# Six of seven groups of streamed tiles begin at other remainders of 256 bytes

## The chip, the cores and the metric

The kernel runs on one core of one Trainium2 chip. The metric is the device time of one launch in microseconds (us). Before the change the median of two runs is 1595.04 us (1594.94 to 1595.14).

## The reference, cut to what matters

There are four batches of 3136 positions. An attention without softmax is followed by a small gated convolution layer, all in float32:

```
scores = (z @ z.T) / 3136                 # z: 3136 x 64
attn   = relu(scores) ** 2
x      = u * (attn @ v)                   # v, u: 3136 x 256
h      = relu(x @ w_in)                   # w_in: 256 x 1024
conv   = sum over k of conv_w[k] * h shifted by k-1 positions, k = 0, 1, 2
out    = (h * sigmoid(conv)) @ w_out      # w_out: 1024 x 256
```

## The kernel before, in words

**Number format.** Every product is made of three matmuls. Each operand is split into a rounded part (`_hi`, in the format that TensorE takes for four-byte operands) and the rest (`_lo`), and hi by hi, lo by hi and hi by lo are summed in PSUM. ScalarE writes each `_hi` tile by a copy, VectorE writes each `_lo` tile by a subtraction, both in the same layout.

**Two kinds of operands.** A matmul has a stationary operand, loaded 128 columns at a time by a weight load (`z_hi`, `z_lo`, `v_hi`, `v_lo`, `w_hi`, `w_lo`), and a moving operand, which streams through the array column by column. Seven groups of tiles stream: `z_mv` (the positions of a block, hi and lo, for the scores), `attn_hi` and `attn_lo` (for attn @ v), `x_hi` and `x_lo` (for x @ w_in), `g_hi` and `g_lo` (for the last product). Every weight load and every matmul of the blocks works on 64 of the 128 partitions, so matmuls come in pairs, one on the upper and one on the lower half, that run side by side. Only the products of the last block use all 128.

**Blocks.** 28 blocks, seven per batch. A block is 448 positions wide in the first three batches, and 512, 512, 512, 448, 448, 448 and 256 in the last. In each block PAIRS = 13 steps go over the keys. A step issues on TensorE, in an order written out by hand: attend for one pair of key tiles (line 481, in two halves), a piece of the up or down product of the block before (lines 503 and 527), the scores three steps ahead (line 397; lines 429, 434 and 437 for the last key tile of a block). Each matmul has its own weight load. The tables USUAL and NARROW say at which step each piece of the layer after the attention is made. The last block's layer stands alone at the end (lines 547 and 567), and the last two blocks keep their gated tiles in the space of `v_hi` and `v_lo`.

**Widths.** Scores, attend and up products stream the block's own width. The down product streams 450 columns in the last block of the first three batches and 258 in the last of all, where the convolution's border belongs to the block.

**Addresses.** Every tensor is laid at a multiple of LINE = 256 bytes. The seven moving groups have SHIFT = 16 elements of four bytes in front, so their first column is 64 bytes past such a multiple. Their rows are PITCH = 512 elements (2048 bytes) apart, so every row begins at the same remainder. The gated tiles in `v_hi` and `v_lo` keep the same 64 bytes (lines 272 to 276), except that the last block's second rows lie 288 elements (1152 bytes) on and so begin at remainder 192. All stationary tiles begin at multiples of 512 bytes. `h_sb`, which VectorE and ScalarE read and write, has rows of 516 elements, so its rows begin at eight different remainders, 16 bytes apart.

**Around the matmuls.** ScalarE makes the first relu of a score tile (line 649), rounds `attn_hi` (658), `x_hi` (675) and `g_hi` (724), and forms `h_sb` (698). VectorE squares (834), subtracts for `attn_lo` (855), `x_lo` (885), `g_lo` (916) and the low half of `z_mv` (934), and makes two taps of the convolution (895, 903). The loads and stores are issued on SyncE's queue and none of them touches a moving tile.

Of the kernel before, what the change touches and what calls it, by code (L numbers as in the profile page):

```python
# [6 lines left out]
F32R = mybir.dt.float32r  # L7
# [3 lines left out]
P = 128  # L11
# [9 lines left out]
PITCH = 512  # L21
# [10 lines left out]
AHEAD = 3  # L32
LINE = 256
SHIFT = 16

RAW = 512
RING = 6
# [81 lines left out]
def program(nc, z_win, z_all, v_all, u_win, w_all, conv_w, out):  # L119
    with ExitStack() as ctx:  # L120
        def sb(name, shape, dt=F32):
            return ctx.enter_context(nc.sbuf_tensor(name, shape, dt, align_bytes=LINE))

        def shifted(name, rows, columns):
            return sb(name, [P, SHIFT + rows * columns], F32R)[:, SHIFT:].rearrange("p (r k) -> p r k", r=rows)

        def sem(name):
            return ctx.enter_context(nc.semaphore(name))
# [1 line left out]

        z_hi = sb("z_hi", [P, PAIRS * P], F32R)
        z_lo = sb("z_lo", [P, PAIRS * P], F32R)
        z_mv = sb("z_mv", [P, SHIFT + 4 * PITCH], F32R)[:, SHIFT:].rearrange("p (b r k) -> p b r k", b=2, r=2)
        z_raw = sb("z_raw", [P, WIDE])
        v_hi = sb("v_hi", [P, TILES * MODEL], F32R)
        v_lo = sb("v_lo", [P, TILES * MODEL], F32R)
# [4 lines left out]

        attn = sb("attn", [P, 3, 2, WIDE])
        attn_hi = shifted("attn_hi", 6, PITCH)
        attn_lo = shifted("attn_lo", 6, PITCH)

        u_sb = sb("u_sb", [P, CM, WIDE])
        x_sb = sb("x_sb", [P, CM, WIDE])
        x_hi = shifted("x_hi", CM, PITCH)
        x_lo = shifted("x_lo", CM, PITCH)
        h_sb = sb("h_sb", [P, FT, HWIDE])  # L150
        g_sb = sb("g_sb", [P, 2, 2, WIDE])
        g_hi = shifted("g_hi", 2, PITCH)
        g_lo = shifted("g_lo", 2, PITCH)
# [116 lines left out]
        def gated_parts(m, F):  # L270
# [4 lines left out]
            at = (FP * 2 * PITCH if m == BLOCKS - 1 else 0) + F * step  # L275
            return [part[:, at:at + step].rearrange("p (r k) -> p r k", r=2)[:, :, SHIFT:] for part in (v_hi, v_lo)]

# [838 lines left out]
```

## Time and profile before

| | us |
|---|---|
| median of the runs | 1595.04 |
| the profiled execution's own time | 1595.02 |
| its span, first to last instruction | 1593.2 |
| TensorE matmul busy | 1584.1 (99%) |
| TensorE weight load busy | 1560.5 (98%) |
| VectorE busy | 1390.5 (87%) |
| ScalarE busy | 1169.3 (73%) |
| GpSimd busy | 35.8 (2%) |

The busy time of TensorE is the time in which at least one matmul was in flight. Since several are in flight at once, the duration of one (359 ns at 448 columns) says little of the rate. The rate is read from the distance between the starts of successive matmuls in the timeline. A timeline line with x2 holds one pair (upper and lower half), a line with x4 two pairs.

### The profile page before, as it was taken

The page shows a single profiled execution, that of the slowest core. Times are in us where ns is not written, and L with a number is a line of the kernel's source. Part 1 is how long each engine was busy: PE and PEld are TensorE (multiplying, and loading weights), DVE is VectorE, ACT ScalarE, POOL GpSimd, SP SyncE. Part 2 cuts the span into 40 slices and gives each one's busy share as a digit, 9 for nine tenths or more (in the row PEclk, how much of TensorE's full clock was granted, in tenths as well). Part 3 has the DMA queues.
Part 4 walks back from the last instruction along what each step waited for, and adds up shares of the span by engine and source line. Part 5 has one row for each costly group of instructions (what it writes and reads, how often), then busy time and mean ns, then how long its engine had stood idle before and what let it go on. Part 6 is the DMA issues. An engine that isn't in the chain of part 4 may idle for free.

```text
span 1593.2 us, 37744 instructions
## 1 busy us (share of the span) xinstructions
PE 1584.1 (99%) x15604; PEld 1560.5 (98%) x15604; DVE 1390.5 (87%) x1940; ACT 1169.3 (73%) x2016; POOL 35.8 (2%) x28
## 2 busy tenths in 40 slices
PE   9999999999999999999999999999999999999998
PEld 7999999999999999999999999999999999999998
DVE  7898888899988888889998888888999888888888
ACT  7777677777777777778777677777877676777776
POOL 6200000000000000000000000000000000000000
PEclk9999999999999999999999999999999999999999
DMA  5100000111000000011200000001110000000000
GB/s 161 38 19 21 23 19 30 53 45 59 22 28 21 31 13 19 30 52 45 65 33 14 19 30 13 19 30 66 52 51 33 4 29 14 19 32 15 21 15 31
DMA packets 29770, 53.16 MB, mean 33 GB/s; under 512 B 2720, under 2 KB 19744, under 8 KB 29600
## 3 DMA queue, kind: packets, MB, share of 16 engines
q1 hardware_dynamic: 29600, 50.76, 9.8%
q8 instruction: 124, 2.03, 0.5%
q14 instruction: 46, 0.38, 0.1%
HBM read 37.89 MB, written 12.85 MB: 32 GB/s over the span
## 4 chain that ended last, share of the span: by engine, by line
PE 95%; DVE 2%; ACT 1%; issue 1%; POOL 0%; DMA 0%; SPq 0%; ACTq 0%
PE ps_av L481 50%; PE ps_h L503 16%; PE ps_y L527 16%; PE ps_s L397 12%; ACT attn_hi L658 0%; POOL v_lo L1061 0%; DVE v_lo L916 0%; DVE attn_lo L855 0%; DMA raw<-v_all 0%; PE ps_s L567 0%; ACT attn L649 0%; DVE g_sb L903 0%; DVE g_sb L895 0%; PE ps_s L429 0%; DVE attn L834 0%
## 5 line engine op out<-in xcount | busy, mean ns | idle before, releaser
L649 ACT ACTIVATE attn<-ps_s 128x448 f32<-128x448 f32 (+2 forms) x650 | 318.4, 542 | 377.5 <-PE ps_s L397 375.9
L834 DVE SCALAR_TENSOR_TENSOR attn<-ps_s,attn 128x448 f32<-128x448 f32 (+2 forms) x650 | 374.9, 618 | 124.2 <-ACT attn L649 122.4
L481 PE MATMUL ps_av<-attn_hi,v_hi 64*128 64x448 f32 (+2 forms) x2740 | 453.9, 359 | 1.1 <-DVE x_sb L879 0.8
L481 PE MATMUL ps_av<-attn_hi,v_lo 64*128 64x448 f32 (+2 forms) x2740 | 454.0, 359 | 0.3 <-POOL v_lo L1061 0.2
L481 PE MATMUL ps_av<-attn_lo,v_hi 64*128 64x448 f32 (+2 forms) x2740 | 453.3, 359 | 0.5 <-DVE attn_lo L855 0.5
L855 DVE TENSOR_TENSOR attn_lo<-attn,attn_hi 128x896 fp32r<-128x896 f32 (+3 forms) x363 | 384.5, 1059 | 55.9 <-ACT attn_hi L658 30.7
L658 ACT ACTIVATE attn_hi<-attn 128x896 fp32r<-128x896 f32 (+3 forms) x363 | 335.9, 925 | 0.1
L481 PEld LDWEIGHTS ps_av<-attn_hi,v_hi 64*128 64x128 f32 x2740 | 326.2, 184 | 5.5 <-issue 2.7
L481 PEld LDWEIGHTS ps_av<-attn_hi,v_lo 64*128 64x128 f32 x2740 | 326.2, 184 | 4.0 <-POOL v_lo L1061 1.6
L481 PEld LDWEIGHTS ps_av<-attn_lo,v_hi 64*128 64x128 f32 x2740 | 326.6, 184 | 3.4 <-DVE attn_lo L855 0.9
L397 PE MATMUL ps_s<-z_mv,z_hi 64*128 64x448 f32 (+2 forms) x1296 | 276.1, 360 | 0.0
L503 PE MATMUL ps_h<-x_hi,w_hi 64*128 64x448 f32 (+1 forms) x864 | 199.9, 363 | 0.4 <-issue 0.2
L503 PE MATMUL ps_h<-x_lo,w_hi 64*128 64x448 f32 (+1 forms) x864 | 199.7, 362 | 0.0
L503 PE MATMUL ps_h<-x_hi,w_lo 64*128 64x448 f32 (+1 forms) x864 | 199.6, 362 | 0.0
L527 PE MATMUL ps_y<-g_lo,w_hi 64*128 64x448 f32 (+2 forms) x832 | 193.8, 363 | 0.0
L527 PE MATMUL ps_y<-g_hi,w_hi 64*128 64x448 f32 (+2 forms) x832 | 193.6, 363 | 0.0
L527 PE MATMUL ps_y<-g_hi,w_lo 64*128 64x448 f32 (+2 forms) x832 | 193.5, 363 | 0.0
L397 PEld LDWEIGHTS ps_s<-z_mv,z_hi 64*128 64x128 f32 x1296 | 178.8, 184 | 2.0 <-DVE attn L834 0.7
L397 PE MATMUL ps_s<-z_mv,z_lo 64*128 64x448 f32 (+2 forms) x648 | 148.3, 359 | 0.0
L895 DVE SCALAR_TENSOR_TENSOR g_sb<-h_sb,taps,g_sb 128x448 f32<-128x448 f32 (+3 forms) x218 | 141.3, 690 | 0.0
L903 DVE SCALAR_TENSOR_TENSOR g_sb<-h_sb,taps,g_sb 128x448 f32<-128x448 f32 (+3 forms) x218 | 140.2, 685 | 0.0
L710 ACT ACTIVATE g_sb<-h_sb,taps 128x448 f32<-128x448 f32 (+3 forms) x218 | 134.4, 669 | 0.0
(133 smaller groups left out, 1898.6 us busy)
## 6 DMA issues: line engine op xcount, KB each, us to landing
raw<-v_all SPq DMA_DIRECT2D x48, 256.0 KB, 2.7
u_sb<-u_win SPq DMA_DIRECT2D x24, 448.0 KB, 3.8
out<-y_sb SPq DMA_DIRECT2D x21, 448.0 KB, 2.9
z_raw<-z_win SPq DMA_DIRECT2D x24, 224.0 KB, 3.7
raw<-z_all SPq DMA_DIRECT2D x12, 256.0 KB, 3.4
raw<-w_all SPq DMA_DIRECT2D x8, 256.0 KB, 2.9
u_sb<-u_win SPq DMA_DIRECT2D x3, 512.0 KB, 3.4
out<-y_sb SPq DMA_DIRECT2D x3, 512.0 KB, 2.6
```

Of the source, the lines that this page charges most:

```text
L397: done = mm(scores_bank(n, p)[:, e, 0:WIDTHS[n]], w[rows, at:at + P], z_mv[rows, n % 2, z, 0:WIDTHS[n]], start=k == 0, stop=k == 2)
L481: done = mm(ps_av[:, c, 0:WIDTHS[n]], v[rows, j * MODEL + c * P:j * MODEL + (c + 1) * P], a[rows, 2 * slot(n, p) + e, 0:WIDTHS[n]], start= ...
L503: done = mm(ps_h[:, e, 0:WIDTHS[m]], w[rows, at:at + P], x[rows, c, 0:WIDTHS[m]], start=k == 0 and not second, stop=k == 3 * CM - 1 and se ...
L527: done = mm(ps_y[:, c, 0:outputs(m)], w[rows, at:at + P], g[rows, e, 0:outputs(m)], start=F == 0 and e == 0 and k == 0 and not second, sto ...
L649: act.activation(attn[:, slot(n, p), e, 0:WIDTHS[n]], scores_bank(n, p)[:, e, 0:WIDTHS[n]], ACT.Relu, scale=1.0 / SEQ / SEQ).then_inc(relu ...
L658: act.activation(attn_hi[:, at:at + k, 0:WIDTHS[n]], attn[:, slot(n, p), 0:k, 0:WIDTHS[n]], ACT.Copy).then_inc(attn_rounded, 1)
L710: act.activation(gated(m, f // 2)[:, f % 2, 0:outputs(m)], h_sb[:, f, 0:outputs(m)], ACT.Copy, scale=taps[:, 0, f:f + 1]).then_inc(tap0_re ...
L834: dve.scalar_tensor_tensor(a, scores_bank(n, p)[:, e, 0:WIDTHS[n]], 0.0, a, ALU.max, ALU.mult).then_inc(attn_ready, 1)
L855: dve.tensor_tensor(attn_lo[:, at:at + k, cols], attn[:, slot(n, p), 0:k, cols], attn_hi[:, at:at + k, cols].bitcast(F32), ALU.subtract).t ...
L895: dve.scalar_tensor_tensor(g, h_sb[:, f, HALO:HALO + outputs(m)], taps[:, 1, f:f + 1], g, ALU.mult, ALU.add).then_inc(tap1_ready, 1)
L903: dve.scalar_tensor_tensor(g, h_sb[:, f, 2 * HALO:2 * HALO + outputs(m)], taps[:, 2, f:f + 1], g, ALU.mult, ALU.add).then_inc(conv_ready, 1)
```

## The change

Each moving group but `attn_hi` gets its own lead in place of the common 16 elements. In bytes: `z_mv` 48, `attn_lo` 80, `x_lo` 96, `g_hi` 160, `x_hi` 192, `g_lo` 224; `attn_hi` stays at 64. The leads are at most 64 elements long, so with the rounding to 256 bytes every tensor keeps its place and only the columns within the six tensors move. The number of instructions, their order and their waits are untouched. The gated tiles inside `v_hi` and `v_lo` still use SHIFT.

```
+SHIFTS = {"x_hi": 48, "x_lo": 24, "g_hi": 40, "g_lo": 56, "attn_lo": 20, "z_mv": 12}
...
         def shifted(name, rows, columns):
-            return sb(name, [P, SHIFT + rows * columns], F32R)[:, SHIFT:].rearrange("p (r k) -> p r k", r=rows)
+            by = SHIFTS.get(name, SHIFT)
+            return sb(name, [P, by + rows * columns], F32R)[:, by:].rearrange("p (r k) -> p r k", r=rows)
...
-        z_mv = sb("z_mv", [P, SHIFT + 4 * PITCH], F32R)[:, SHIFT:].rearrange("p (b r k) -> p b r k", b=2, r=2)
+        z_mv = sb("z_mv", [P, SHIFTS["z_mv"] + 4 * PITCH], F32R)[:, SHIFTS["z_mv"]:].rearrange("p (b r k) -> p b r k", b=2, r=2)
```

## Rows read from the trace of the kernel before

**Rows 1.** The page: busy time by engine, granted clock in 40 slices, chain by engine.

```profile
PE 1584.1 (99%) x15604; PEld 1560.5 (98%) x15604; DVE 1390.5 (87%) x1940; ACT 1169.3 (73%) x2016; POOL 35.8 (2%) x28
...
PEclk9999999999999999999999999999999999999999
...
PE 95%; DVE 2%; ACT 1%; issue 1%; POOL 0%; DMA 0%; SPq 0%; ACTq 0%
```

**Rows 2.** The page's groups: busy us, mean ns | idle before, what ended it.

```profile
L481 PE MATMUL ps_av<-attn_lo,v_hi 64*128 64x448 f32 (+2 forms) x2740 | 453.3, 359 | 0.5 <-DVE attn_lo L855 0.5
...
L397 PE MATMUL ps_s<-z_mv,z_hi 64*128 64x448 f32 (+2 forms) x1296 | 276.1, 360 | 0.0
L503 PE MATMUL ps_h<-x_lo,w_hi 64*128 64x448 f32 (+1 forms) x864 | 199.7, 362 | 0.0
...
L397 PE MATMUL ps_s<-z_mv,z_lo 64*128 64x448 f32 (+2 forms) x648 | 148.3, 359 | 0.0
```

**Rows 3.** TensorE's groups by shape, lines 527 and 437.

```profile
L527 PE MATMUL ps_y<-g_lo,w_hi 64*128 64x448 f32 x640 | 143.0, 358 | 0.0
...
L527 PE MATMUL ps_y<-g_lo,w_hi 64*128 64x450 f32 x96 | 25.7, 365 | 0.0
...
L527 PE MATMUL ps_y<-g_lo,w_hi 64*128 64x512 f32 x96 | 25.0, 389 | 0.0
...
L437 PE MATMUL ps_s<-z_mv,z_lo 64*128 64x448 f32 x24 | 8.6, 359 | 0.0
```

**Rows 4.** Timeline of TensorE, 448 columns: start us, length us, instruction.

```profile
764.17 0.46 PE L503 MATMUL ps_h<-x_hi,w_hi 64*128 64x448 f32 x2
...
765.37 0.46 PE L397 MATMUL ps_s<-z_mv,z_hi 64*128 64x448 f32 x2
...
767.17 0.66 PE L481 MATMUL ps_av<-attn_hi,v_hi 64*128 64x448 f32 x4
```

**Rows 5.** Timeline of TensorE, last pairs of a stretch of 450 columns.

```profile
422.59 0.40 PE L527 MATMUL ps_y<-g_hi,w_lo 64*128 64x450 f32 x2
422.79 0.40 PE L527 MATMUL ps_y<-g_hi,w_hi 64*128 64x450 f32 x2
423.00 0.40 PE L527 MATMUL ps_y<-g_lo,w_hi 64*128 64x450 f32 x2
423.21 0.40 PE L527 MATMUL ps_y<-g_hi,w_lo 64*128 64x450 f32 x2
```

**Rows 6.** Timeline of TensorE, 512 columns, ten pairs apart.

```profile
1306.37 0.66 PE L481 MATMUL ps_av<-attn_hi,v_hi 64*128 64x512 f32 x4
...
1308.66 0.66 PE L481 MATMUL ps_av<-attn_lo,v_hi 64*128 64x512 f32 x4
```

**Rows 7.** Timeline of TensorE, 256 columns in two stretches, ten pairs apart each.

```profile
1534.41 0.42 PE L481 MATMUL ps_av<-attn_hi,v_hi 64*128 64x256 f32 x4
...
1535.59 0.42 PE L481 MATMUL ps_av<-attn_lo,v_hi 64*128 64x256 f32 x4
...
1544.37 0.42 PE L481 MATMUL ps_av<-attn_hi,v_hi 64*128 64x256 f32 x4
...
1545.51 0.42 PE L481 MATMUL ps_av<-attn_lo,v_hi 64*128 64x256 f32 x4
```

**Rows 8.** Timeline of TensorE, last block: third, seventh and twelfth matmul of twelve.

```profile
1582.32 0.28 PE L567 MATMUL ps_s<-v_hi,w_lo 128*128 128x258 f32 x1
...
1582.80 0.28 PE L567 MATMUL ps_s<-v_hi,w_hi 128*128 128x258 f32 x1
...
1583.40 0.28 PE L567 MATMUL ps_s<-v_hi,w_lo 128*128 128x258 f32 x1
```

**Rows 9.** ScalarE's groups by shape: tiles written at one remainder, and at eight.

```profile
L649 ACT ACTIVATE attn<-ps_s 128x448 f32<-128x448 f32 x554 | 271.4, 542 | 318.5 <-PE ps_s L397 317.0 <-PE ps_s L418 1.4
...
L698 ACT ACTIVATE h_sb<-ps_h 128x448 f32<-128x448 f32 x192 | 94.3, 544 | 3.0
```

## The prediction

> **What bounds the kernel now.** I read the busy shares and the chain of waits first [rows 1]: TensorE is busy 99% of the span, the chain that ended last lies on it for 95%, and its granted clock is in the top tenth in every slice, that is, the 2.4 GHz level. The groups [rows 2] show that it hardly waits: 0.5 us ahead of the 2740 matmuls that stream attn_lo, and nothing ahead of those on z_mv and x_lo. So the time is the number of pairs of matmuls times the distance between their starts: 15604 / 2 = 7802 pairs, which at 200 ns would be 1560 us of the 1593.2. Whatever changes that distance changes the time, and whatever changes only VectorE or ScalarE changes it little.
>
> Then I read the distance in the timeline. At 448 columns, 15 pairs lie between the starts 764.17 and 767.17 [rows 4]: **200 ns a pair**, alike in three products with different tiles. At 512 columns ten pairs take 2.29 us, 229 ns each [rows 6]; at 256 columns they take 1.14 us or 1.18 us, 114 or 118 ns [rows 7]. One column at 2.4 GHz is 0.417 ns, so the columns alone would need 187, 213 and 107 ns. The excess is 13, 16 and 7 ns: it grows with the length of the stream and isn't a fixed price of a matmul. Something rations the stream by pieces of it.
>
> The third reading is the one that the forecast rests on. A stretch of 450 columns starts at the usual distance and then settles to 0.20, 0.21 and 0.21 us [rows 5]; from 422.59 to 423.21 it is 0.62 / 3 = 207 ns. Two columns more cost about **7 ns**, where two columns of array time are 0.8 ns. And 200 / 28 = 7.1 ns, where 28 is the number of 16-column pieces (64 bytes) in 448; 229 / 32 is 7.2, 114 / 16 is 7.1, and 207 / 29 is 7.1. The stream is delivered in pieces of 64 bytes, and a piece of which only two columns are wanted costs as much as a whole one.
>
> **The change, part by part.** No instruction, wait, DMA or order changes, and no tensor moves; only the first byte of six moving groups. The open point is whether those 64-byte pieces lie on fixed addresses. All streams of before begin at 64 bytes past 256, or at 192, so the trace can't say. I take it that they do, because a memory's pieces usually have places, and price it from [rows 5]. It is a choice, and its other answers are the rivals.
>
> Then a stream of 448 columns that begins 48, 80 (16), 96 (32), 160 (32) or 224 (32) bytes into its grid touches 29 pieces in place of 28, and one of 512 touches 33 in place of 32. Each costs 7 ns a pair.
>
> - attn_lo, remainder 80: 2740 matmuls [rows 2], 1370 pairs, 9.6 us.
> - z_mv, remainder 48: 1296 + 648 matmuls [rows 2], 972 pairs, and three lines of which one has 24 matmuls of 448 [rows 3], about 40 pairs more: 1012 pairs, 7.1 us.
> - x_lo, remainder 96: 864 matmuls [rows 2], 432 pairs, 3.0 us.
> - g_hi and g_lo, remainders 160 and 224: per part 640 matmuls of 448 and 96 of 512 [rows 3], three parts, (640 + 96) x 3 / 2 = 1104 pairs, 7.7 us. The 450-column ones cost nothing more: 32 bytes into a piece, 450 columns end 8 + 450 = 458 columns on, still in the 29th piece.
> - x_hi, remainder 192: a multiple of 64 bytes, nothing. The last block supports that: its first gated row begins at 64 and its second at 192, and the distance is 0.12 us in both, 0.48 us for four starts and 0.60 us for five [rows 8]. If it did cost 7 ns, 864 x 2 / 2 pairs would add 6.0 us.
> - The full-height matmuls of the last block that stream x_lo number 16: 0.1 us, left out.
> - Writes by VectorE and ScalarE at new remainders: ScalarE writes h_sb rows that begin at eight remainders 16 bytes apart in 544 ns, and attn rows at aligned places in 542 ns [rows 9]. So 0 to 2 ns an instruction. What hides it is VectorE's idle 13%, 203 us [rows 1]: even 100 ns on each of some 500 split instructions, 50 us, would leave it under TensorE; uncovered, that would be late split tiles and waits ahead of line 481. A slower TensorE gives these engines more room.
>
> Sum: 3918 pairs x 7 ns = **27.4 us**. On the profiled execution's own 1595.02 us, which is within 0.1 us of the median, that makes **1622 us**, 1.7% more. Nothing stands ready to absorb it, since TensorE is the bound throughout.
>
> Both ends of the unknown price: upward, the extra piece at the start and one at the end each count, 14 ns a pair, 55 us. Downward, the excess over the columns' own time, 13 ns at 448 [rows 4], could vanish for all six groups: 3918 + 864 pairs x 13 ns = 62 us less. I take 7, the value measured for a partly used piece in the same instruction form.
>
> **Rivals.**
>
> *The pieces are counted from the operand's own start (no effect).* Then 450 columns are 29 pieces and 448 are 28, wherever they begin: [rows 5] fit as well, and [rows 8] too. All new remainders are multiples of 16 bytes, so a grid of 16 bytes comes to the same. Time 1595 us. The change would move bytes and do nothing to the time. The Trainium skill, "SBUF — State Buffer", section "Door 1: The DMA port swizzle", says that the memory has lines of 16 bytes and that accesses pay when they cross into a new line; by that rule no stream here touches one line more, and the time stays. What no run here shows yet is that line size; the 7 ns for two more columns speaks for pieces of four such lines.
>
> *A grid of 32 bytes.* Only the remainders 48 and 80 are off it: z_mv and attn_lo, 2382 pairs, 16.7 us at the same price, 1612 us. Against it: 450 columns would be 57 half-pieces, 3.6 ns more, and I read 7.
>
> *Staggering helps (faster).* If the excess of 13 ns comes from streams, weight loads and writes of other engines meeting because all begin at like places, then different remainders might break it. For it: 256 columns show two rates, 114 and 118 ns, in stretches with the same addresses [rows 7], so meeting in time does matter to some nanoseconds. Against: the 448-column streams hold 200 ns in all products, whatever else runs. All of it back is 1533 us; half of it, 31 us, is 1564 us and about the 2% line. The Trainium skill, "TensorE: Matmul & The Clock Gate", section "Back-to-back issue gap", gives N / 2.4 + 2.5 ns for a single warm matmul, 189 ns at 448 columns; the trace's 200 disagrees. By that figure 11 ns a pair are there to be won, 53 us on the six groups.
>
> *The sequence breaks (slower by over 2%).* Now each stream ends where the next one begins, modulo 256 bytes: 448, 512 and 256 columns are whole multiples of 256 bytes. With different remainders that no longer holds between attn_hi and attn_lo, x_hi and x_lo, g_hi and g_lo. If a jump costs as much as a piece beside the extra piece itself, it is 14 ns a pair: 3918 x 14 = 55 us, 1650 us. For it: after a stretch of 450 columns, whose end is off the next start, the distance is 7 ns up. It decides from 31.9 us / 3918 = 8.1 ns a pair on, only 1.1 ns over my price, and x_hi's 6.0 us would do it too.
>
> **Numbers.** The forecast (64-byte grid, all five groups at about 7 ns, 1615 to 1632) gets 0.36; no effect 0.25; the 32-byte grid 0.05; the broken sequence 0.17; staggering 0.17. A measurement of this kernel tells about 2% from no change. The forecast's own spread puts a fifth of its 0.36 over the 2% line at 1627; of staggering's 0.17 about 0.12 lies over 2%. So faster 0.12, slower 0.17 + 0.07 = 0.24, the same 0.64. The range has to hold 8 in 10: 1572 (a third or so of staggering's gain) to 1652 (the broken sequence's 1650), which leaves out most of staggering and a few cases above.
>
> **What would show it.** In the timeline after, the distance between pairs that stream attn_lo, z_mv, x_lo and g settles to 207 ns and stays at 200 for attn_hi and x_hi, averaged over a run of them, since the rate seems to answer a few matmuls late. Attend, which is two parts attn_hi and one part attn_lo, would average 202.3 ns; scores 207; up 202.3; down 207. The 450-column stretches would not change. Matmul counts, clock and waits stay. 1595 throughout means the start doesn't matter; z_mv and attn_lo alone at 207 means 32 bytes; an effect in attn_hi's or x_hi's pairs means that it isn't the count of pieces.

## The result, and the profile after

The changed kernel takes **1608.36 us** (1608.29 to 1608.43, two runs) against 1595.04 us: ratio 1.0081, 95% interval 1.0065 to 1.0097. It is 13.3 us slower, half of the 27.4 us that the prediction's sum gave. The span of the profiled execution is 1606.5 us. The time given for a kernel is the median of its executions at the full granted clock; one execution of e15 (below), at 0.869 of it, took 1716.6 us and is left out.

The page of the changed kernel, with the same three lines as [rows 1]:

```profile
PE 1596.8 (99%) x15604; PEld 1555.6 (97%) x15604; DVE 1391.3 (87%) x1940; ACT 1169.6 (73%) x2016; POOL 35.8 (2%) x28
...
PEclk9999999999999999999999999999999999999999
...
PE 95%; DVE 2%; ACT 1%; issue 1%; POOL 0%; DMA 0%; SPq 0%; ACTq 0%
```

Counts, clock and chain are the same. VectorE and ScalarE are busy as long as before to within 1 us in all, so their writes at new remainders cost nothing that shows; TensorE has 12.7 us more. Its groups, which answer to [rows 2]:

```profile
L483 PE MATMUL ps_av<-attn_lo,v_hi 64*128 64x448 f32 (+2 forms) x2740 | 463.5, 360 | 0.6 <-DVE attn_lo L857 0.6
...
L399 PE MATMUL ps_s<-z_mv,z_hi 64*128 64x448 f32 (+2 forms) x1296 | 282.5, 361 | 0.0
L505 PE MATMUL ps_h<-x_lo,w_hi 64*128 64x448 f32 (+1 forms) x864 | 206.7, 367 | 0.0
...
L399 PE MATMUL ps_s<-z_mv,z_lo 64*128 64x448 f32 (+2 forms) x648 | 153.3, 361 | 0.0
```

No wait was added: 0.6 us ahead of attn_lo, nothing ahead of the others. The matmuls themselves come at a greater distance. A stretch of 600 us, all of it at 448 or 450 columns, gives that as a count. The columns are the stretch, its length, and for TensorE, weight loads, VectorE, ScalarE and GpSimd the busy time and the count, then clock, DMA share and GB/s. The kernel before:

```profile
200.00:800.00 600.00, 599.85 (x5991) 598.72 (x5989) 532.11 (x746) 445.02 (x766) 0.00 (x0) 1.00 0.11 36
```

The changed kernel:

```profile
200.00:800.00 600.00, 599.96 (x5945) 590.63 (x5943) 527.67 (x739) 441.65 (x760) 0.00 (x0) 1.00 0.11 35
```

600 us over half of 5991 is 200.3 ns a pair before, and over half of 5945 it is 201.9 ns after. Times 7802 pairs, the difference is 12.1 us, nearly all of the change. I use this count for every kernel below and call it the rate.

The timeline of TensorE in the changed kernel shows where in a step it lies:

```profile
301.12 0.43 PE L529 MATMUL ps_y<-g_hi,w_hi 64*128 64x448 f32 x2
...
302.35 0.62 PE L483 MATMUL ps_av<-attn_hi,v_hi 64*128 64x448 f32 x4
...
303.55 0.42 PE L505 MATMUL ps_h<-x_hi,w_hi 64*128 64x448 f32 x2
...
304.77 0.42 PE L399 MATMUL ps_s<-z_mv,z_hi 64*128 64x448 f32 x2
...
305.38 0.62 PE L483 MATMUL ps_av<-attn_hi,v_hi 64*128 64x448 f32 x4
```

Six pairs on g take 1.23 us (205 ns each), six of attend 1.20 us (200), six on x 1.22 us and three on z_mv 0.61 us (203), where [rows 4] has 200 for attend, up and scores.

One cycle, read to 10 ns, can't tell a nanosecond a pair. So here is the mean over all matmuls of 448 columns that start between 200 and 1150 us: the distance from a start to the next start on the same row half, by product, in ns.

| | attend | up (x) | scores (z_mv) | down (g) |
|---|---|---|---|---|
| kernel before | 200.1 | 200.0 | 200.2 | 200.1 |
| changed kernel | 200.6 | 203.0 | 202.4 | 203.7 |

With 4110 pairs of attend (2740 x 3 / 2), 1296 of up, 1012 of scores and 1104 of down, that is 2.1 + 3.9 + 2.2 + 4.0 = 12.2 us, an estimate that gives the 448-column rate to all widths. Attend, for which I had priced the largest term, pays 2 us.

### The profile page after: what moved, and what is told of

It is laid out like the page before. It is cut to its first block, busy times and chain, and to the rows that moved or that the text cites. A ratio compares the mean times of both kernels' runs of the same rounds, so it can differ in the third digit from the quotient of the medians.

```text
span 1606.5 us, 37744 instructions
## 1 busy us (share of the span) xinstructions
PE 1596.8 (99%) x15604; PEld 1555.6 (97%) x15604; DVE 1391.3 (87%) x1940; ACT 1169.6 (73%) x2016; POOL 35.8 (2%) x28
## 4 chain that ended last, share of the span: by engine, by line
PE 95%; DVE 2%; ACT 1%; issue 1%; POOL 0%; DMA 0%; SPq 0%; ACTq 0%
PE ps_av L483 50%; PE ps_h L505 17%; PE ps_y L529 16%; PE ps_s L399 12%; ACT attn_hi L660 0%; POOL v_lo L1063 0%; DVE v_lo L918 0%; DMA raw<-v_all 0%; DVE attn_lo L857 0%; PE ps_s L569 0%; ACT attn L651 0%; DVE g_sb L905 0%; DVE g_sb L897 0%; PE ps_s L439 0%; PE ps_s L436 0%
## 5 line engine op out<-in xcount | busy, mean ns | idle before, releaser
L483 PE MATMUL ps_av<-attn_hi,v_hi 64*128 64x448 f32 (+2 forms) x2740 | 463.4, 360 | 1.0 <-DVE x_sb L881 0.8
L483 PE MATMUL ps_av<-attn_lo,v_hi 64*128 64x448 f32 (+2 forms) x2740 | 463.5, 360 | 0.6 <-DVE attn_lo L857 0.6
L483 PE MATMUL ps_av<-attn_hi,v_lo 64*128 64x448 f32 (+2 forms) x2740 | 461.8, 359 | 0.2
L483 PEld LDWEIGHTS ps_av<-attn_hi,v_hi 64*128 64x128 f32 x2740 | 334.7, 184 | 8.9 <-issue 2.5
L483 PEld LDWEIGHTS ps_av<-attn_hi,v_lo 64*128 64x128 f32 x2740 | 333.6, 184 | 7.1 <-POOL v_lo L1063 1.5
L483 PEld LDWEIGHTS ps_av<-attn_lo,v_hi 64*128 64x128 f32 x2740 | 333.0, 184 | 6.7 <-DVE attn_lo L857 0.9
L399 PE MATMUL ps_s<-z_mv,z_hi 64*128 64x448 f32 (+2 forms) x1296 | 282.5, 361 | 0.0
L505 PE MATMUL ps_h<-x_lo,w_hi 64*128 64x448 f32 (+1 forms) x864 | 206.7, 367 | 0.0
L505 PE MATMUL ps_h<-x_hi,w_lo 64*128 64x448 f32 (+1 forms) x864 | 205.7, 365 | 0.0
L529 PE MATMUL ps_y<-g_hi,w_lo 64*128 64x448 f32 (+2 forms) x832 | 199.4, 366 | 0.0
```

The source lines that it names most:

```text
L399: done = mm(scores_bank(n, p)[:, e, 0:WIDTHS[n]], w[rows, at:at + P], z_mv[rows, n % 2, z, 0:WIDTHS[n]], start=k == 0, stop=k == 2)
L483: done = mm(ps_av[:, c, 0:WIDTHS[n]], v[rows, j * MODEL + c * P:j * MODEL + (c + 1) * P], a[rows, 2 * slot(n, p) + e, 0:WIDTHS[n]], start= ...
L505: done = mm(ps_h[:, e, 0:WIDTHS[m]], w[rows, at:at + P], x[rows, c, 0:WIDTHS[m]], start=k == 0 and not second, stop=k == 3 * CM - 1 and se ...
L529: done = mm(ps_y[:, c, 0:outputs(m)], w[rows, at:at + P], g[rows, e, 0:outputs(m)], start=F == 0 and e == 0 and k == 0 and not second, sto ...
```

## The experiments

**Is there a grid of 64 bytes?** Four kernels, in which only the leads differ. In the first three all seven groups share one; in the fourth the six lie on the grid, at 128 or 192 bytes, and attn_hi stays at 64.

```
-SHIFT = 16
+SHIFT = 20      # e1: 80 bytes. e2: 24 (96 bytes). e3: 0
...
 # e4, with SHIFT = 16
+SHIFTS = {"x_hi": 48, "x_lo": 32, "g_hi": 32, "g_lo": 48, "attn_lo": 32, "z_mv": 48}
```

> All seven moving groups begin at remainder 80, attn_hi included; nothing else differs from the kernel before. Fixed 64-byte places, priced from the change itself (13.3 us over 3918 pairs, 3.4 ns a pair): every one of some 7600 pairs of 448, 512 or 256 columns touches one piece more, so 26 us, 1621 us (at the 7 ns of the prediction 53 us, 1648 us). Jumps between different starts: there are none, as before, so 1595 us. If 64 itself is a favoured remainder, anything above 1595.

> All seven moving groups begin at remainder 96. Fixed 64-byte places: as at 80, 1621 us (or 1648). A grid of 32 bytes: 1595 us while 80 is slow. Jumps between different starts: none, 1595 us.

> All seven moving groups begin at remainder 0, where the stationary tiles begin too. Fixed 64-byte places: 1595 us, since 0 lies on the grid. Jumps: 1595 us. If the common start with the weight loads costs anything, it is over 1595 here alone.

> The six groups begin at different remainders that all lie on the 64-byte grid: z_mv 192, attn_lo 128, x_lo 128, g_hi 128, x_hi 192, g_lo 192, attn_hi 64. Fixed 64-byte places: no stream touches a piece more, 1595 us. Jumps between different starts: of the order of 3000 pairs follow one on another remainder; if these made the 13.3 us of the change (4.4 ns each), the time is about that of the change, 1608 us.

| | us | ratio to before, 95% interval |
|---|---|---|
| e1, all at 80 | 1625.9 | 1.0186 (1.0170 to 1.0202) |
| e2, all at 96 | 1631.9 | 1.0230 (1.0214 to 1.0245) |
| e3, all at 0 | 1629.8 | 1.0216 (1.0201 to 1.0232) |
| e4, on the grid at 64, 128 and 192 | 1609.4 | 1.0090 (1.0073 to 1.0106) |

The same 600 us of e3, all at 0:

```profile
200.00:800.00 600.00, 600.00 (x5817) 563.31 (x5817) 516.45 (x722) 432.05 (x744) 0.00 (x0) 1.00 0.11 35
```

And of e4, on the grid:

```profile
200.00:800.00 600.00, 600.00 (x5941) 599.23 (x5940) 527.02 (x739) 441.38 (x759) 0.00 (x0) 1.00 0.11 35
```

With everything at 0, on the grid, the rate is 206.3 ns and the kernel 34.5 us slower. In e4 no stream touches a further 64 bytes and yet it costs as much as the change (202.0 ns). **The grid of 64 bytes falls**, and "no effect" with it. So does the thought that jumps between unlike starts are the only price: e1 to e3 have none. 64 is simply a good common start.

e1 shows one thing more. Its four executions span 1621.1 to 1627.3 us, and within the profiled one the rate isn't steady:

```profile
200.00:700.00 500.00, 500.00 (x4919) 497.20 (x4918) 433.58 (x606) 361.75 (x623) 0.00 (x0) 1.00 0.09 30
850.00:1150.00 300.00, 300.00 (x2906) 277.52 (x2905) 250.97 (x348) 208.32 (x358) 0.00 (x0) 1.00 0.08 26
```

The start is 80 bytes throughout, and the pairs come at 203.3 ns first and at 206.5 ns later. In the second stretch the two row halves no longer run as pairs (a row half is the upper or the lower 64 partitions). At 1001.9 us one half begins its first matmul on g, while the other has two more to do on attn_lo before it gets there:

```profile
1001.89 0.36 PE L529 MATMUL ps_y<-g_hi,w_hi 64*128 64x448 f32 x1
1001.93 0.36 PE L483 MATMUL ps_av<-attn_lo,v_hi 64*128 64x448 f32 x1
```

So what the other half does at the time may matter too. No run tests that, and a rate below can depend on the stretch as well as on the start.

**The stream's own address, or its distance to the weight loads?** All stationary tensors begin at 0 in the kernels so far. Here a lead of 64 bytes stands ahead of all six, and they follow each other without rounding (each is a multiple of 256 bytes long).

```
+        lead = sb("lead", [P, 16])
+        z_hi = ctx.enter_context(nc.sbuf_tensor("z_hi", [P, PAIRS * P], F32R, align_bytes=64))
...      # z_lo, v_hi, v_lo, w_hi, w_lo likewise; the gated rows inside v_hi, v_lo begin at SHIFT - 16
 # e5: SHIFT = 16, streams at 64.  e6: SHIFT = 32, streams at 128
```

> All six stationary tensors begin at remainder 64 in place of 0, all seven moving groups stay at 64, so both begin alike as in the run with everything at 0. If the distance between the two starts decides (a stream and the weight load of the next matmul meet in the memory): the rates of the run with everything at 0, 206.7 ns a pair at 448 columns, about 1630 us. If the stream's own address decides: 200 ns and 1595 us.

> Stationary tensors at remainder 64, moving groups at 128: the distance of 64 of the kernel before, at other addresses. If the distance decides: 200 ns a pair, 1595 us. If the stream's own address decides: whatever 128 gives by itself, and unless 128 is as good as 64, above 1595 us.

e5: 1630.8 us, ratio 1.0220 (1.0205 to 1.0235). Its 600 us:

```profile
200.00:800.00 600.00, 600.00 (x5810) 579.22 (x5808) 515.76 (x722) 431.31 (x743) 0.00 (x0) 1.00 0.11 35
```

e6: 1595.3 us, ratio 0.9999 (0.9989 to 1.0009). Its 600 us:

```profile
200.00:800.00 600.00, 599.84 (x5991) 596.70 (x5990) 531.96 (x746) 444.99 (x766) 0.00 (x0) 1.00 0.11 36
```

This is the clearest pair of the study. Streams at 64 are slow (206.5 ns) as soon as the weights are at 64 too, and streams at 128 are as fast as before, to the last matmul of 5991, when the weights are 64 behind. The tensors lie in the same order in e5 and e6, so the new order isn't the cause. **With a common start, the distance between streams and weights decides, and not the streams' own place**: so it is at both distances that were tried, 0 and 64 bytes. That they can meet is plain from the loads' timeline of the kernel before, in the same stretch as [rows 4]:

```profile
764.17 0.29 PEld L503 LDWEIGHTS ps_h<-x_lo,w_hi 64*128 64x128 f32 x2
```

The load for the next pair starts with the stream of this one, and 184 ns of the 200 are load.

**The map of common starts.** Three kernels, run once each. Every moving tile of block n begins OFF[n] elements into its row; OFF changes every three blocks of the first three batches, where the width leaves room for it (the list is written short here).

```
+OFF = [16] * 3 + [0] * 3 + [32] * 3 + [48] * 3 + [8] * 3 + [24] * 3 + [40] * 3 + [0] * 7      # e7
...
-                                      a[rows, 2 * slot(n, p) + e, 0:WIDTHS[n]],
+                                      a[rows, 2 * slot(n, p) + e, OFF[n]:OFF[n] + WIDTHS[n]],
...      # and so for z_mv, x and g, where they are written and where they are read
```

> All seven moving groups begin at one common remainder, which changes every three blocks of the first three batches: 64, 0, 128, 192, 32, 96, 160 bytes; the last batch at 0. Stationary tensors at 0. Known: 64 gives 200.0 ns a pair at 448 columns, 0 gives 206.7 ns, 96 gives 205.3 ns. A fixed grid of 64 bytes: 0, 64, 128, 192 alike, which the run with everything at 0 already speaks against. Distance to the weight loads: each remainder has a rate of its own between 193 and 207 ns, steady within its blocks.

> As the sweep before, at the remainders 16, 48, 80, 112, 144, 176, 224 bytes. Known: 80 gives 203.3 or 206.7 ns a pair. If only places of 64 bytes mattered, the off-grid ones would all lie above their neighbours on the grid; if the distance to the weight loads counts in whole pieces, they lie between or at their neighbours.

> Common remainders of 208, 240, 8, 24, 56, 72, 168 bytes, three blocks each, the last batch at 0. If the distance to the weight loads decides, each has a rate of its own, and 8, 24, 56, 72 and 168 lie near those of the multiples of 16 beside them (0 or 16, 16 or 32, 48 or 64, 64 or 80, 160 or 176). So far the best are 200 ns (64, 16, at times 160) and the worst 206.7. A remainder with a rate under 200 ns would give a kernel faster than the one before.

The windows below lie in the last two of three blocks. e7, at 0, 192, 32 and 160 bytes:

```profile
216.00:328.00 112.00, 112.00 (x1091) 103.56 (x1089) 93.61 (x130) 77.85 (x134) 0.00 (x0) 1.00 0.11 36
...
560.00:670.00 110.00, 110.00 (x1092) 110.00 (x1090) 93.56 (x130) 77.90 (x134) 0.00 (x0) 1.00 0.07 22
732.00:843.00 111.00, 111.00 (x1082) 109.74 (x1080) 102.57 (x147) 85.23 (x150) 0.00 (x0) 1.00 0.14 43
...
1077.00:1186.00 109.00, 109.00 (x1089) 108.60 (x1086) 98.54 (x139) 82.45 (x142) 0.00 (x0) 1.00 0.17 53
```

e8, at 48, 80 and 112 bytes:

```profile
217.00:328.00 111.00, 111.00 (x1097) 111.00 (x1096) 94.90 (x131) 78.06 (x135) 0.00 (x0) 1.00 0.10 36
388.00:499.00 111.00, 111.00 (x1091) 108.61 (x1089) 98.20 (x138) 81.19 (x142) 0.00 (x0) 1.00 0.08 25
560.00:671.00 111.00, 111.00 (x1079) 110.95 (x1078) 93.21 (x129) 76.65 (x132) 0.00 (x0) 1.00 0.06 22
```

e17, at 24, 56, 72 and 168 bytes:

```profile
562.00:674.00 112.00, 112.00 (x1091) 111.96 (x1090) 93.89 (x130) 77.91 (x134) 0.00 (x0) 1.00 0.06 22
735.00:847.00 112.00, 112.00 (x1100) 109.95 (x1097) 103.43 (x147) 86.90 (x152) 0.00 (x0) 1.00 0.14 45
908.00:1021.00 113.00, 113.00 (x1091) 112.96 (x1089) 94.35 (x130) 77.88 (x135) 0.00 (x0) 1.00 0.06 21
1081.00:1193.00 112.00, 112.00 (x1115) 110.86 (x1113) 100.59 (x141) 84.65 (x146) 0.00 (x0) 1.00 0.18 56
```

Window over half the count gives the rates; a matmul that is only partly inside is counted, so against the starts themselves they are 0.5 to 0.9 ns low.

| common start, bytes | ns a pair | | ns a pair |
|---|---|---|---|
| 0 | 205.3 | 160 | 200.2 |
| 32 | 205.2 | 168 | 200.9 |
| 48 | 202.4 | 176 | 203.5 |
| 80 | 203.5 | 192 | 201.5 |
| 96 | 204.8 | 208 | 202.2 |
| 112 | 205.7 | 224 | 204.2 |
| 128 | 203.3 | 240 | 202.2 |
| 144 | 205.7 | 24 | 205.3 |
| 8 | 205.1 | 56 | 203.6 |
| | | 72 | 207.1 |

64, 16 and 208 ran as the first three blocks, with shorter windows: from 105 to 157 us of e7 524 matmuls are counted, from 102 to 157 us of e8 552 and of e17 544, that is 198.5, 199.3 and 202.2 ns. So short a window is 1 to 2 ns low; by the starts themselves the three have 200.2, 200.3 and 204.0 ns. The map is no grid and has no slope: 16, 64 and 160 are good, 0 and 32 on either side of 16 are bad. Its period isn't 128 bytes, since 32 and 160 differ by 5 ns; that it is 256 is taken from how the tensors lie, and no run had a lead of 256 or more. Each value is one stretch of one execution, and e1 shows how far a stretch can stray: 3 ns. Nothing beats 64, so no better version came of it. e17's expectation for 8, 24, 56 and 72 held in part: 8 and 24 go with 0 and 32, not with 16 between them, and 72 is worse than both 64 and 80.

**Do the parts of the change add?** Kernels with one part of it, and two with attn_lo elsewhere.

```
 # e9, e10, e11: attn_lo at 0, 16, 80 bytes
+SHIFTS = {"attn_lo": 0}      # 4 in e10, 20 in e11
 # e12
+SHIFTS = {"x_hi": 48, "x_lo": 24, "g_hi": 40, "g_lo": 56}
 # e16
+SHIFTS = {"z_mv": 12}
```

> Only attn_lo moves, to remainder 0; the other six groups stay at 64. If each stream costs what its own distance to the weight loads costs, whatever its neighbours do: 1370 pairs at 206.7 in place of 200 ns, 9.1 us, 1604.6 us. If a change of start from one stream to the next makes the cost (some 1200 of them here, at the 13.3 us / 3000 of the change): 5 us, and the same with attn_lo at 16 or at 80.

> Only attn_lo moves, to remainder 16, which by the sweep is as good as 64 (200 ns). Own distance decides: 1595.5 us. A change of start between neighbours: 1600 us, as with attn_lo at 0.

> One part of the change alone: attn_lo at 80. Own distance, by the sweep's 203.0 to 205.1 ns: 1370 pairs at 3 to 5 ns, 4 to 7 us, 1600 to 1602 us. The prediction's step: 9.6 us, 1605 us.

> The x and g parts of the change alone: x_hi 192, x_lo 96, g_hi 160, g_lo 224. Own distance, by the sweeps: x_hi 864 pairs at 2.2 ns, x_lo 432 at 5.3, g_hi 736 at 0.7, g_lo 368 at 4, 6.1 us, 1601.4 us. The prediction's steps: x_hi nothing, the rest 10.7 us, 1606 us.

> One part of the change alone: z_mv at 48. The parts measured so far are attn_lo at 80, 2.2 us, and x and g together, 11.8 us. If the parts add to the 13.3 us of the change, z_mv costs -0.7 us, 1594.5 us. By the sweep's rate for a common start of 48 it costs 2.9 us, 1598 us, and the parts then sum to 17, more than the whole. The prediction's step: 7.1 us, 1602 us.

| | us | more than before | ratio, 95% interval |
|---|---|---|---|
| e9, attn_lo at 0 | 1603.4 | 8.3 | 1.0050 (1.0035 to 1.0065) |
| e10, attn_lo at 16 | 1603.9 | 8.7 | 1.0052 (1.0037 to 1.0067) |
| e11, attn_lo at 80 | 1597.4 | 2.2 | 1.0013 (1.0003 to 1.0022) |
| e12, x and g | 1607.0 | 11.8 | 1.0071 (1.0054 to 1.0088) |
| e16, z_mv | 1597.8 | 2.6 | 1.0018 (1.0009 to 1.0027) |

e10 decides. 16 is as good a common start as 64, so by the theory of own distances attn_lo at 16 is free; it costs 8.7 us, as much as at 0. Its timeline:

```profile
305.81 0.59 PE L483 MATMUL ps_av<-attn_hi,v_hi 64*128 64x448 f32 x4
...
307.02 0.60 PE L483 MATMUL ps_av<-attn_hi,v_hi 64*128 64x448 f32 x4
...
308.24 0.39 PE L505 MATMUL ps_h<-x_hi,w_hi 64*128 64x448 f32 x2
...
309.44 0.39 PE L399 MATMUL ps_s<-z_mv,z_hi 64*128 64x448 f32 x2
```

The first six pairs of attend take 1.21 us, the second six 1.22 us, and the next six on x_hi and x_lo, which all begin at 64, 1.20 us. The means over 200 to 1150 us, taken as above, in ns:

| | attend | up (x) | scores (z_mv) | down (g) |
|---|---|---|---|---|
| e10, attn_lo at 16 | 201.8 | 200.9 | 200.4 | 200.9 |
| e11, attn_lo at 80 | 200.6 | 200.1 | 200.2 | 200.2 |
| e12, x and g | 200.2 | 203.9 | 201.6 | 204.7 |
| e16, z_mv | 200.1 | 200.0 | 202.2 | 200.1 |

Of e10's 8.7 us about 7 are attend's (4110 pairs at 1.7 ns), where the starts alternate, and the rest lies in up and down, whose tiles didn't move. In e12 scores pay 1.4 ns, though z_mv didn't move. So a stream's time hangs on more than its own start. And one price for every change of start, the other theory, fails as well: e9, e10 and e11 have the same changes at the same places and cost 8.3, 8.7 and 2.2 us. Neither rule holds alone. The parts of the change, 2.2 + 11.8 + 2.6 = 16.6 us, are more than the whole, 13.3 us: scores pay 1.4 ns in e12 and 2.0 ns in e16 but only 2.2 ns in the whole change, and up and down pay about 1 ns less in the change than in e12. The rates of the map would give 4.8 us for attn_lo (1370 pairs at 3.5 ns), 6.1 us for x and g (e12's expectation) and 2.9 us for z_mv (e16's), 13.8 us in all. That this is near the change is a coincidence: measured alone, the first is 2.2 us and the second 11.8 us.

**The change moved as a whole.** e18 is the change with stationary tensors and all streams 64 bytes further.

```
+        lead = sb("lead", [P, 16])      # and the stationary tensors behind it, as in e5
-SHIFT = 16
+SHIFT = 32
+SHIFTS = {"x_hi": 0, "x_lo": 40, "g_hi": 56, "g_lo": 8, "attn_lo": 36, "z_mv": 28}
```

> The change with everything that TensorE reads moved on by 64 bytes: stationary tensors at 64, and attn_hi 128, z_mv 112, attn_lo 144, x_lo 160, g_hi 224, x_hi 0, g_lo 32. If only distances between streams and loads (and between successive streams) decide, its cost is the change's, 1608.4 us. If the streams' own remainders decide, as in the sweeps, x_hi at 0 and g_lo at 32 are among the dearest and x_lo at 160 among the cheapest, and the sum of the common-start rates is 1617 us: attn_hi 2740 pairs at 3.9 ns, attn_lo 1370 at 6.4, z_mv 1012 at 6.5, x_hi 864 at 6.7 and the g pair at 4 to 6 would give even 1630 us.

1607.7 us, ratio 1.0075 (1.0058 to 1.0091), and in its 600 us

```profile
200.00:800.00 600.00, 599.97 (x5943) 594.86 (x5942) 527.59 (x739) 441.69 (x760) 0.00 (x0) 1.00 0.11 35
```

5943 matmuls against the change's 5945. So with mixed starts too, a move of everything that TensorE reads by 64 bytes changes nothing: the distances count, not the places.

**Is it the length of the weight load?** A guess at the mechanism: a stream loses 6.7 ns each time it meets the load that runs beside it, so a shorter load should be met less. Every matmul that neither opens nor closes a sum gets fewer columns of weights. These kernels leave out those terms in the upper rows of the outputs, so they serve for their times alone.

```
-            mm = nc.tensor.matmul
+            def mm(out, w, x, start, stop):
+                if not (start or stop):
+                    out, w = out[0:96], w[:, 0:96]      # 64 in e14; e15 has SHIFT = 0
+                return nc.tensor.matmul(out, w, x, start=start, stop=stop)
```

> All starts as before the change (64). Every weight load that neither opens nor closes a sum loads 96 columns in place of 128 (the outputs of the upper 32 columns lack those terms); the streams keep their 448 columns. If the 13.3 ns over the columns' own time are the stream meeting the weight load, two meetings of 6.7 ns each in a load of 128 columns, a shorter load is met less often: 1.5 times, 196.7 ns a pair, on some 6900 pairs, 23 us less, 1572 us. If the excess belongs to the stream alone: 1595 us.

> As the run with 96 columns, with 64 columns a load (the upper half of the outputs lacks those terms). Meetings with the load: one in place of two, 193.3 ns a pair, 46 us less, 1549 us. Stream alone: 1595 us. If a narrower load changes the array's arrangement and drains it each time, well above 1595 us, and nothing follows.

> Everything at remainder 0 (1629.8 us with full loads, three meetings a stream) and loads of 96 columns as above. Meetings: 2 to 2.3 in place of 3, 200 to 202 ns, 1595 to 1605 us. Stream alone: 1630 us.

The loads did become shorter. e13, loads of 96 columns:

```profile
L382 PEld LDWEIGHTS ps_av<-attn_hi,v_hi 64*96 64x96 f32 x2688 | 289.8, 158 | 23.9 <-PE ps_av L382 0.5 <-issue 0.2
```

e14, loads of 64 columns:

```profile
L382 PEld LDWEIGHTS ps_av<-attn_hi,v_hi 64*64 64x64 f32 x2688 | 254.2, 131 | 36.1 <-PE ps_av L382 0.5 <-issue 0.3
```

158 and 131 ns against 184 for 128 columns in the kernel before:

```profile
L481 PEld LDWEIGHTS ps_av<-attn_hi,v_hi 64*128 64x128 f32 x2740 | 326.2, 184 | 5.5 <-issue 2.7
```

But e13 takes 1616.4 us (ratio 1.0131, 1.0116 to 1.0146), e14 1603.6 us (1.0049, 1.0032 to 1.0065), e15 1613.6 us (1.0115, 1.0099 to 1.0132). From starts at 64 less loading makes the kernel slower, by 21 us and by 8 us; from starts at 0, where it took 1629.8 us, 96 columns make it 16 us faster. **The guess falls**: there is no price per meeting that falls with the load's length. What stays is that the narrower matmuls move the rate both ways. That doesn't single out the load: the same edit also halves or cuts by a quarter the rows of the output that a matmul writes, and it mixes two widths in one kernel. With 96 columns the two starts differ by 3 us, with 128 by 35. Loads of 128 columns are 512 bytes, those of 64 are 256 and those of 96 are 384, so only the last end off a multiple of 256; but e14 is slower than before as well, and no run tells what makes the difference.

## Why the prediction was wrong

**The step that failed** is the one that the prediction called its choice: that the pieces of 64 bytes lie on fixed addresses, so that a start off that grid costs one piece, 7 ns a pair. What the runs showed in its place: no such grid (everything at 0, on it, costs 34.5 us; e4, on it, costs 14.2 us), but a cost that hangs on the distance between the streams' and the weights' starts (206.5 ns a pair at distance 0, 200.3 at 64, wherever they lie), and with mixed starts on the neighbours too. The range held and the cost was 13.3 us in place of 27.4 us. That the direction came out is luck: 64 bytes happened to be one of the three best common starts, so nearly any move from it costs.

- *The bound, the rate of 200 ns, no new wait:* right. The time is 7802 pairs times their distance, before and after.
- *The excess over the columns' time belongs to the length of the stream:* right as a reading [rows 4, 6, 7], but I took it for a property of the stream alone. At least the part above 200 ns isn't: e5 and e6 differ only in the distance to the weights, 206.5 against 200.3 ns. What the first 13 ns are, no run tells; no start that I tried gets below them at 448 columns.
- *Two more columns cost 7 ns [rows 5]:* measured, but it says nothing of where a stream begins. I used the price of a length for a start.
- *The rates to look for, attend 202.3, scores 207, up 202.3, down 207:* the trace has 200.6, 202.4, 203.0 and 203.7.
- *attn_lo, 9.6 us:* 2.2 us by itself (e11).
- *z_mv, 7.1 us:* 2.6 us (e16).
- *x_hi nothing, x_lo and g 10.7 us:* together 11.8 us (e12), close in size, wrong in reason: e4 puts every stream on the grid and the total is as large. [Rows 8] could not show that x_hi is free; it compares two starts in full-height matmuls of 258 columns only.
- *The 32-byte grid:* against it stand 160 and 96, at 200.2 and 204.8 ns. *No effect:* refuted by any of e1 to e3. *The broken sequence,* 14 ns a pair and 1650 us: too dear, though its idea that a stream feels the one before it would fit e10. *Staggering helps:* no mixture that I ran was faster than the common start at 64.
- *VectorE and ScalarE pay 0 to 2 ns for odd starts:* right, their busy times moved by under 1 us.

The Trainium skill's lines of 16 bytes ("SBUF — State Buffer", "Door 1: The DMA port swizzle") would by themselves have had all the change's starts alike, and the map disagrees: multiples of 16 run from 200 to 206 ns. Starts inside such a line agree with it in part: 72 bytes gave 207.1 ns, where 64 and 80 gave 200 and 203.5 ns, but 168 with 200.9 ns lies between 160 and 176.

**What stays open:** the rule behind the map, how a stream's cost depends on the streams around it, and what the other row half does to it. Shown are two partners (the stream and the weights, e5 and e6), that a shift of both by 64 bytes changes nothing (e6, e18), that streams of unlike starts don't count one by one (e10, e12), and the size, 0 to 8 ns a pair. The previous stream and the other row half are only likely partners.

## What to carry to other kernels

When TensorE is the bound and every matmul brings its own weight load, measure the distance between matmul starts against columns over the clock; an excess of some per cent can hang on where the streamed tile begins relative to the stationary one, within 256 bytes. Give all streamed tiles one common lead and sweep that lead in one kernel, block by block, before anything finer: here it was worth 35 us of 1595 between 0 and 64 bytes. Don't carry the price of a longer operand over to a shifted one, and don't trust a sum that fits the whole until a part has been tested.

## What the runs showed that I had not expected

- The same code with different leads spans 1595 to 1632 us, at the full clock and with hardly a wait more: on no page does a group of TensorE's matmuls wait 2 us in all.
- The best lead depends on the width. A stretch of 82 us, all at 512 columns and at the same point of the work, in the kernel before, in e3 (all at 0) and in e5 (all at 64):

```profile
1266.00:1348.00 82.00, 82.00 (x720) 82.00 (x718) 69.06 (x86) 57.14 (x88) 0.00 (x0) 1.00 0.06 23
1298.00:1380.00 82.00, 82.00 (x727) 82.00 (x725) 69.58 (x86) 58.01 (x89) 0.00 (x0) 1.00 0.06 23
1299.00:1381.00 82.00, 82.00 (x727) 82.00 (x726) 69.60 (x86) 57.93 (x89) 0.00 (x0) 1.00 0.06 23
```

  Here a distance of 0 to the weights is the better one, 225.6 against 227.8 ns a pair (both about 1 ns low), while at 448 columns it is the worse by 6 ns. e5 agrees with e3, so at this width too it is the distance.
- Less work can take longer: 96 in place of 128 columns of weights cost 21 us.
